# The start of a three-part attention and feed-forward kernel: the first block's loads, matrices, new states and layout put in another order

## The reference

```
# r, k, v: (batch 4, heads 8, seq 768, head_dim 48); w, u: (8, 48)
state = zeros(B, H, D, D)
for t in range(S):
    cur      = outer(u * k[t], v[t])
    y[t]     = r[t] @ (state + cur)
    state    = w * state + outer(k[t], v[t])
x = y arranged as (3072 tokens, 384)
h = relu(x @ w_in); x2 = (h * h) @ w_down            # 384 -> 2048 -> 384
out = ((x2 @ w_a) * (x2 @ w_b)) @ w_out              # 384 -> 1536 -> 384
```

## Time and profile before

| | |
|---|---|
| median of 3 runs | 972.02 us (970.56 to 972.78) |
| the profiled execution's own time | 973.94 us |
| its span | 972.2 us |
| TensorE busy (matmul) | 948.9 us, 98% of the span |
| VectorE, ScalarE, GpSimd busy | 398.8, 291.0, 129.4 us |
| granted TensorE clock, mean | 0.992 |

### The profile page before, as it was taken

How to read it: one execution, slowest core, us unless ns; L and a number is a source line. 1 busy time by engine, 2 the same in 40 slices (tenths; PEclk the granted TensorE clock), 3 DMA queues, 4 the chain that set the end, 5 groups by cost and what they waited for, 6 DMA issues and landing times.

```text
span 972.2 us, 16724 instructions
## 1 busy us (share of the span) xinstructions
PE 948.9 (98%) x7231; PEld 802.3 (83%) x7231; DVE 398.8 (41%) x571; ACT 291.0 (30%) x499; POOL 129.4 (13%) x124
## 2 busy tenths in 40 slices
PE   7899999999999999999999999999999999999997
PEld 6777787888788888888888888888888888888886
DVE  5378755556545636443563222222222222222221
ACT  2343432333333233324553222222222222222221
POOL 5235333224222403100000000000000000000000
PEclk9799999999999999999999999999999999999999
DMA  9454636203221430001431002002002001000001
GB/s 147 85 115 102 117 91 108 50 18 80 31 55 48 53 65 34 19 17 66 122 98 65 1 1 65 0 1 66 1 1 65 1 1 40 27 1 20 13 1 33
DMA packets 105688, 46.71 MB, mean 48 GB/s; under 512 B 78221, under 2 KB 104078, under 8 KB 105614
## 3 DMA queue, kind: packets, MB, share of 16 engines
q1 hardware_dynamic: 92048, 39.34, 18.4%
q10 hardware_dynamic: 13566, 6.30, 3.0%
HBM read 32.25 MB, written 9.44 MB: 43 GB/s over the span
## 4 chain that ended last, share of the span: by engine, by line
PE 93%; issue 2%; DVE 1%; ACTq 1%; ACT 1%; DMA 0%; POOL 0%; DVEq 0%; POOLq 0%
PE banks L711 10%; PE banks L712 10%; PE banks L710 10%; PE banks L604 8%; PE banks L605 7%; PE banks L608 7%; PE banks L588 6%; PE banks L589 6%; PE banks L590 6%; PE banks L726 5%; PE banks L725 5%; PE banks L729 5%; PE banks L535 2%; PE banks L478 2%; PE banks L503 1%
## 5 line engine op out<-in xcount | busy, mean ns | idle before, releaser
L1086 DVE TENSOR_TENSOR g_raw<-banks,g_raw 128x512 f32<-128x512 f32 x72 | 49.8, 692 | 284.6 <-PE banks L712 284.6
L711 PE MATMUL banks<-xT,weights 128*128 128x512 f32 x360 | 141.3, 393 | 0.0
L712 PE MATMUL banks<-xT,weights 128*128 128x512 f32 x360 | 141.1, 392 | 0.0
L710 PE MATMUL banks<-xT,weights 128*128 128x512 f32 x360 | 140.4, 390 | 0.0
L1007 DVE TENSOR_TENSOR g_lo<-g_raw,g_hi 128x512 fp32r<-128x512 f32 x96 | 81.9, 854 | 112.1 <-ACT g_hi L756 112.1
L604 PE MATMUL banks<-g_hi,weights 128*128 128x512 f32 x288 | 118.7, 412 | 0.0
L588 PE MATMUL banks<-xT,weights 128*128 128x512 f32 x288 | 113.0, 392 | 3.2 <-DVE weights L310 2.9
L605 PE MATMUL banks<-g_hi,weights 128*128 128x512 f32 x288 | 112.7, 391 | 0.0
L756 ACT ACTIVATE g_hi<-g_raw 128x512 fp32r<-128x512 f32 x96 | 60.7, 633 | 172.9 <-PE banks L608 162.9
L589 PE MATMUL banks<-xT,weights 128*128 128x512 f32 x288 | 112.3, 390 | 0.0
L590 PE MATMUL banks<-xT,weights 128*128 128x512 f32 x288 | 112.3, 390 | 0.0
(11 more groups left out here) (119 smaller groups left out, 1306.2 us busy)
## 6 DMA issues: line engine op xcount, KB each, us to landing
x_dram<-x SPq DMA_DIRECT2D x6, 768.0 KB, 3.2
xT<-x_dram SPq DMA_DIRECT2D x6, 768.0 KB, 5.2
rkv<-in_v SPq DMA_DIRECT2D x22, 192.0 KB, 5.2
result<-x SPq DMA_DIRECT2D x20, 192.0 KB, 2.9
stage<-in_moe_w_out SPq DMA_DIRECT2D x15, 192.0 KB, 3.0
xT<-y_pad SPq DMA_DIRECT2D x20, 144.0 KB, 2.7
stage<-in_moe_w_out ACTq DMA_DIRECT2D x13, 192.0 KB, 2.7
rkv<-in_k SPq DMA_DIRECT2D x12, 192.0 KB, 3.9
```

The lines of the kernel that those rows point to most:

```text
L710: nc.tensor.matmul(dst, hi, xT[:, q, HI, kt, :], start=(kt == 0), stop=False)
L711: nc.tensor.matmul(dst, hi, xT[:, q, LO, kt, :], start=False, stop=False)
L712: last = nc.tensor.matmul(dst, lo, xT[:, q, HI, kt, :], start=False, stop=(kt == KT - 1))
```

## The change

The change rewrites the order of the first block only; the loops over the later blocks stay. In words:

- SP issues the loads of `k` and `r` of the first half, then of the second, then both loads of `v`, then weight tiles 0 and 1. Before, SP issued `k`, `k`, `v` of the first half and the weight tiles, and ACT issued `r`, `r`, `v` of the second half and weight tile 2. ACT now issues only the loads of `w` and `u` at the start.
- SP then issues `repack(sp, 0)`, the six DMAs that lay out y of units 0 and 1, waits until all four units of y are gathered (`y_mixed` at 4), and only then issues weight tiles 2 and 3 and the loads of units 4 to 7.
- The diagonal matrices: units 0 and 2 on ACT, unit 1 on VectorE (one instruction), unit 3 on GpSimd.
- GpSimd starts `k_times_u` after VectorE's tables are made (`tables_made`), not when `u_rows` are there.
- TensorE: `renew_state` of units 0 and 1 stands after the gathering of y of both units and after `take_y` of its unit; `place_x` is called for units 2 and 3 only. 12 warming transposes in two groups of 6 take the place of 8 in one.
- `take_y` of unit 2 and 3 waits for the landed `repack(0)`, which reads the `y_pad` columns that it overwrites. `x_hi` and `x_lo` of units 0 and 1 read the landed copies.

```
--- before.py
+++ after.py
...
     RKV = 2 * (2 * RK + DM) + HP - D
     RK_LOADS, V_LOADS = 16 * 3, 16 * 2
     HI, LO = 0, 1
-    WARM_START, WARM_TURNS = 8, 8
+    WARM_START, WARM_TURNS = 8, 6
     assert B == 4 and BT == 512 and H * D == DM and KT == PAIRS - 1
     assert 2 * RKV >= LATE * 2 * W2 and (N2 - LATE) * 2 * W2 <= N1 * 2 * W1
...
         def placed(e):
-            return bank[UNITS + e][:, 0:DM].rearrange("p (k t) -> p k t", k=KT)
+            return bank[2 + e][:, 0:DM].rearrange("p (k t) -> p k t", k=KT)
+        def matrix_of(e):
+            return (eye[:, :].unsqueeze(1).unsqueeze(1).broadcast_to([P, 2, PAIRS, T]),
+                    diag[:, e % 2, :, :].rearrange("p g q -> p q g").unsqueeze(3).broadcast_to([P, 2, PAIRS, T]))
         x2_dram = nc.dram_tensor("x2_dram", [BLOCKS, P, KT * BT], F32, kind="Internal").ap()
         in_main = w_in[0:KT * MAIN, :].rearrange("(k p) f -> p k f", k=KT)
...
         scored, masked = sem("scored"), sem("masked")
         w_turned, u_spread, u_made = sem("w_turned"), sem("u_spread"), sem("u_made")
         diag_made, pad_made = sem("diag_made"), sem("pad_made")
-        matrices_made, last_matrix_made = sem("matrices_made"), sem("last_matrix_made")
+        matrices_made, odd_matrices_made = sem("matrices_made"), sem("odd_matrices_made")
         scores_ready, y_mixed, mixed = sem("scores_ready"), sem("y_mixed"), sem("mixed")
         ku_made, rku_made, k_tail_made = sem("ku_made"), sem("rku_made"), sem("k_tail_made")
         decay_made, state_made, state_read = sem("decay_made"), sem("state_made"), sem("state_read")
...
             return min(e, LEAVING)
         def half_landed(eng, e):
-            eng.wait_ge(x_landed[e // 2 % 2], REPACK * (e // UNITS))
+            eng.wait_ge(x_landed[e // 2 % 2], REPACK * (e // UNITS + (1 if e % UNITS < 2 else 0)))
         def half_loaded(eng, loaded, e):
             eng.wait_ge(loaded[e // 2 % 2], (V_LOADS if loaded is v_loaded else RK_LOADS) * (e // UNITS + 1))
...
                 sp.dma_start(xT[:, n % 2, LO, :, :].rearrange("p k t -> p (k t)").bitcast(F32),
                              x2_dram[n, :, :]).then_inc(x2_loaded[n % 2], 16)
-            load_rk(sp, 0, 1, k, k_loaded)
-            load_rk(sp, 2, 1, k, k_loaded)
-            load_v(sp, 0)
+            for e in (0, 2):
+                load_rk(sp, e, 1, k, k_loaded)
+                load_rk(sp, e, 0, r, r_loaded)
+            for e in (0, 2):
+                load_v(sp, e)
             load_weights(sp, 0)
             load_weights(sp, 1)
+            repack(sp, 0)
+            sp.wait_ge(y_mixed, UNITS)
+            load_weights(sp, 2)
+            load_weights(sp, STAGES)
             load_half(UNITS)
-            load_weights(sp, STAGES)
             load_half(UNITS + 2)
             for n in range(BLOCKS):
...
                     diag[:, e % 2, :, :].rearrange("p g q -> p q g").unsqueeze(3)
                     .broadcast_to([P, 2, PAIRS, T]), ALU.mult).then_inc(pad_made, 1)
+            def odd_matrix(e):
+                pool.wait_ge(diag_made, e + 1)
+                nc.gpsimd.tensor_tensor(pad_early[e], *matrix_of(e), ALU.mult).then_inc(odd_matrices_made, 1)
             pool.wait_ge(u_made, 1)
+            pool.wait_ge(tables_made, 1)
             for e in range(2):
                 k_times_u(e)
             for e in range(2):
                 times_r(e)
-            pool.wait_ge(pow_raw_made, 1)
             nc.gpsimd.tensor_tensor(tail_pow_t, pow_raw[:, :, ::-1],
                                     w_pow2[:, 5, :, :].rearrange("p g i -> p (g i)").unsqueeze(2)
                                     .broadcast_to([P, 2 * PAIRS, T]), ALU.mult).then_inc(tail_pow_made, 1)
...
                 k_times_u(e)
             pool.wait_ge(tail_made, 1)
             tail(0)
-            tail(1)
             for e in range(2, UNITS):
                 times_r(e)
-            pool.wait_ge(diag_made, UNITS)
-            nc.gpsimd.tensor_tensor(
-                pad_early[3], eye[:, :].unsqueeze(1).unsqueeze(1).broadcast_to([P, 2, PAIRS, T]),
-                diag[:, 1, :, :].rearrange("p g q -> p q g").unsqueeze(3).broadcast_to([P, 2, PAIRS, T]),
-                ALU.mult).then_inc(last_matrix_made, 1)
+            tail(1)
+            odd_matrix(3)
             tail(2)
             tail(3)
             decay(2)
...
             def first_scores(e):
                 half_loaded(pe, v_loaded, e)
                 pe.wait_ge(masked, e + 1)
-                if e < UNITS - 1:
-                    pe.wait_ge(matrices_made, e + 1)
-                else:
-                    pe.wait_ge(last_matrix_made, 1)
+                pe.wait_ge((matrices_made, odd_matrices_made)[e % 2], e // 2 + 1)
                 mix_scores(e)
             def place_x(e):
...
                 pe.wait_ge(y_made, e + 1)
                 cols = slice(e % 2 * P, (e % 2 + 1) * P)
                 for kt in range(KT):
-                    to = bank[UNITS + e][:, kt * P:(kt + 1) * P]
+                    to = bank[2 + e][:, kt * P:(kt + 1) * P]
                     nc.tensor.matmul(to, choose_own[0:PR], y_pad[0:PR, kt, cols], start=True, stop=False)
                     last = nc.tensor.matmul(to, choose_last[kt][0:PR], y_pad[0:PR, KT, cols], start=False, stop=True)
                 last.then_inc(x_placed, 1)
...
             turn_r(0)
             turn_r(1)
+            pe.wait_ge(u_made, 1)
+            free = [bank[1][:, j * P:(j + 1) * P] for j in range(4)]
+            warm(WARM_TURNS, free)
             pe.wait_ge(table_step, 1)
             turn_k(2)
             turn_k(3)
+            warm(WARM_TURNS, free)
             score(0)
+            score(1)
+            turn_r(2)
             pe.wait_ge(tail_pow_made, 1)
             for g in range(PAIRS):
                 last = nc.tensor.transpose(bank[3][:, g * P:(g + 1) * P],
                                            g_flat[:, BT + g * P:BT + (g + 1) * P], ident[:, :])
             last.then_inc(tail_turned, 1)
-            score(1)
-            pe.wait_ge(u_made, 1)
-            warm(WARM_TURNS, [bank[1][:, j * P:(j + 1) * P] for j in range(4)])
-            turn_r(2)
             pe.wait_ge(tail_made, 1)
             turn_r(3)
-            for e in range(2):
-                first_scores(e)
-                renew_state(e)
+            first_scores(0)
+            first_scores(1)
+            pe.wait_ge(y_made, 1)
+            renew_state(0)
             score(2)
             score(3)
             mix_state(2)
+            pe.wait_ge(y_made, 2)
+            renew_state(1)
             first_scores(2)
+            mix_state(3)
+            first_scores(3)
             pe.wait_ge(choice_made, 3)
-            place_x(0)
-            mix_state(3)
-            place_x(1)
-            first_scores(3)
             place_x(2)
             place_x(3)
             for e in range(2, UNITS):
                 renew_state(e)
             up(0, 0)
...
             def take_y(e):
                 act.wait_ge(y_mixed, e + 1)
-                if UNITS + 2 > e >= 2:
-                    act.wait_ge(x_placed, e - 1)
+                if UNITS <= e < UNITS + 2:
+                    act.wait_ge(x_placed, e - UNITS + 1)
                 elif e >= 2:
                     half_landed(act, e - 2)
-                if e < LEAVING and not 2 <= e < UNITS:
+                if UNITS <= e < LEAVING:
                     act.wait_ge(mixed, e + 1)
                 y = both(banks_of(e), 0, PAIRS * T)[0:PR].rearrange("p i (g t) -> p i g t", g=PAIRS)
                 to = y_pad[0:PR, :, e % 2 * P:(e % 2 + 1) * P].rearrange("p g (i t) -> p i g t", i=2)
                 nc.scalar.activation(to, y, ACT.Copy).then_inc(y_made, 1)
             def first_x_hi(e):
-                act.wait_ge(x_placed, e + 1)
+                act.wait_ge(x_placed, e - 1)
                 nc.scalar.activation(xT[:, 0, HI, :, cols_of(e)], placed(e), ACT.Copy).then_inc(x_hi_made, 1)
             def x_hi(e):
...
             act.dma_start(w_rows.rearrange("g (q d) -> g q d", q=2)[:, :, 0:D], w.rearrange("(g q) d -> g q d", q=2))\
                 .then_inc(w_loaded, 16)
             act.dma_start(u_row.rearrange("p (h d) -> p h d", h=H), u.unsqueeze(0)).then_inc(u_loaded, 16)
-            load_rk(act, 0, 0, r, r_loaded)
             act.wait_ge(u_spread, 1)
             nc.scalar.activation(u_rows[:, :, :].rearrange("p h d -> p (h d)"), bank[1][:, 0:DM], ACT.Copy)\
                 .then_inc(u_made, 1)
-            load_rk(act, 2, 0, r, r_loaded)
-            load_v(act, 2)
-            load_weights(act, 2)
-            act.wait_ge(tail_turned, 1)
-            nc.scalar.activation(tail_pow[:, :, :], bank[3][:, :].rearrange("p (h d) -> p h d", h=H)[:, :, 0:D],
-                                 ACT.Copy).then_inc(tail_made, 1)
             def make_matrices(e):
                 act.wait_ge(diag_made, e + 1)
                 for h in range(H):
...
             act.wait_ge(masks_made, 6)
             make_matrices(0)
```

(49 more changed lines are left out.)

## The result

The changed kernel took 966.24 us in the median of 4 executions (964.5 to 966.75), the kernel before 972.4 (970.56 to 973.01). The ratio is 0.9937, with a 95% interval of 0.9918 to 0.9955: 6.1 us less. Six more executions of it, measured later, had a median of 965.44 against 972.84 for 17 of the kernel before: 0.992 (0.9901 to 0.9939), 7.4 us less. The direction was as forecast; the forecast was 961.5, a gain of 10.5, with a range that ended at 965.5. The time lies 0.7 us outside it.

The account below looks back on a forecast made before the run. TensorE bounds, so `up(0, 0)` starting earlier is the gain: 5.8 + 1.4 + 1.8 + 1.0 (earlier start) + 0.5 (shorter gaps) = 10.5, taking 973.94 to 963.4, 961.5 as median. Range 959.5 to 963.5; 8 in 10, 957.5 to 965.5.

Parts of the forecast that it names:

- The tables at 0.69 each: VectorE's two table products: with GpSimd held back, 0.69 us each instead of 1.37 and 1.48.
- the chain through mask, sum, matrices and `tail_pow`: From `score(0)` at 14.1 through VectorE and ScalarE: `first_scores(0)` at 19.2 instead of 20.21, gaining only 1.0 us.
- the 150 GB/s of the forecast: Rate assumed for the early loads in one queue: `v` lands at 16.9 and 19.5, weight tiles by 24.
- 44.82 - 34.3 = 10.5: Start of `up(0, 0)` before, less its forecast start after: the whole gain, 10.5 us.
- One of the two issue waits stays, 1.0, and the one under the loads goes, since these now wait: TensorE between the first gatherings and `place_x(2)`: one wait of 1.0 us left, ending the second road at 30.0.
- the issue wait 1.8: Term of the sum: 1.8 us saved by losing the idle wait in `first_scores(2)`, during which loads ran.
- the rival to which I gave 0.10 at 964.5: Clock falls to 0.50 on the placing, which costs 3.0 us more: gain 7.5, 964.5 us; chance 0.10.
- two `place_x` at low clock 5.8: Term of the sum: dropping the placing of units 0 and 1 from TensorE saves 5.8 us.
- the low clock on what stood between and behind them 1.4: Term of the sum: work between and behind the two dropped placings escapes the low clock, saving 1.4 us.
- The waits for weights in the first steps stay as they were: Behind `up(0, 0)`, layer one: weight tile 2 lands at 34.5, just in time for its split; no added wait.
- The rival on the slower side: Held-back loads of units 4 and 5 starve layer one: 981 us at 50 GB/s; chance 0.03.
- The better rival: Before `up(0, 0)`, clock and queue run better, without issue waits: gain 13 to 14, 958.5 us; chance 0.25.

Follow-up runs that it names:

- again_2: The changed kernel with no edit, one single execution for a third trace: 966.61 us, no ratio.
- fill: The changed kernel with 14 more warming transposes ahead of the turning of `tail_pow`: 965.65 us, ratio 0.9926 to the kernel before.
- sums_first: The changed kernel with VectorE's diagonal sums of units 0 and 1 and unit 1's matrix ahead of unit 0's mask: 964.74 us, ratio 0.9915.
- pool_wait: The changed kernel with GpSimd starting `k_times_u(4)` only when the rest of weight tile 3 is made: 964.89 us, ratio 0.9912.
- pool_early: The changed kernel with GpSimd started when `u_rows` are there, beside VectorE's tables, as before: 965.84 us, ratio 0.992.
- more_code: The changed kernel with 32 tiny 4-column transposes in front of the turning of `tail_pow`, where TensorE waits: 966.63 us, ratio 0.9928.
- place_all: The changed kernel with `place_x` on TensorE for all four units and no `repack(0)`: 966.99 us, ratio 0.9937.
- again: The changed kernel with no edit, executed six more times: 965.44 us median, ratio 0.992 to the kernel before.
- again_3: The changed kernel with no edit, one single execution for a fourth trace: 964.9 us, no ratio.
- best_a: The changed kernel without the 12 warming transposes and with GpSimd's `k_times_u(4)` held until weight tile 3's rest is made: 963.03 us, ratio 0.9892.
- best_b: As best_a, with the sums of units 0 and 1 ahead of the mask as well: 962.18 us, ratio 0.9885.
- no_warm: The changed kernel without its 12 warming transposes (`WARM_TURNS` from 6 to 0): 962.94 us, ratio 0.9891.

## Why the prediction was wrong

**Right.** What bounds the kernel, and that all hangs on the start of `up(0, 0)`: the rest is 927.1 to 927.7 in six of the eight traces of the two kernels, 928.2 and 928.8 in two. The tables at 0.69 each, hidden; the matrix on VectorE (1.19 us) hidden; the chain through mask, sum, matrices and `tail_pow`, which put `first_scores(0)` at 19.2 (19.4 in the mean of four traces); loads of `r` near 9. The loads themselves were faster than the 150 GB/s of the forecast: 143 to 199 in stretches of 2 us between 5 and 17, through the one queue. That cost the forecast nothing, since no gathering waited for `v`.

**The step that failed** is the sum "44.82 - 34.3 = 10.5", at both ends: the mean start moved by 8.3.

The larger error is the start after, 34.3 against a mean of 35.74, 1.4 us. Up to `first_scores(0)` it is 0.2, and from `place_x(2)` to `up(0, 0)` another 0.2 (4.5 us and not 4.3). The other 1.1 lies between, where 10.8 us were forecast and 11.2 to 11.4 measured in three traces, 13.7 in again_2. The text there says "One of the two issue waits stays, 1.0, and the one under the loads goes, since these now wait". It was the other way round: the wait in the middle of `first_scores(2)`, the one under the loads, stayed in all four traces, with 1.14 to 2.23 us, though the loads were held back; the one in the scores was gone in three of four and 0.46 in the fourth. So 1.6 us of such waits are left in the mean and not 1.0. All waits for "issue" together fell by 1.8 in the mean (3.4 to 1.6), which is the sum's term "the issue wait 1.8"; with its reason, the loads, unsupported, that is luck. The rest is again_2's clock at 0.50 on the last gathering and the placing, the rival to which I gave 0.10 at 964.5. On the placing it held in one of four traces of the changed kernel; fill, sums_first, pool_wait, pool_early and more_code show it too.

The base is 0.8 too high. I measured the change from 44.82, a start that held 9.85 us of low clock; the starts before are 42.36 to 45.36, mean 44.04, since the low stretch ends at 36 in one execution and at 41 in another. The terms "two `place_x` at low clock 5.8" and "the low clock on what stood between and behind them 1.4" count that clock as part of what the change removes. At full clock the two placings cost 3.0 us, by place_all's trace. Then the full 10.5 was taken from the median: "the profiled execution has 973.94, 1.9 above the median; 963.4 there is 961.5 as a median".

**The third error** is "The waits for weights in the first steps stay as they were": 0.4 us in the mean, and against the first trace 1.5 in again and 0.8 in again_3, because the held-back load of unit 4 released GpSimd's product onto VectorE's products there. The Trainium skill, "SBUF — State Buffer", section "Summary: rules for kernel authors", says that the two block each other; I had weighed that on the tables and the matrix only. The traces agree: 1.75 us instead of 0.95 in again, 1.50 instead of 0.69 in again_3.

Together 0.8, 1.4 and 0.4 are 2.6, and 10.5 less 2.6 is the 7.9 of the means, near the 7.4 of the larger measurement. The four executions of each kernel that the forecast was held against give 6.2; the other 1.2 is their scatter. So is the side of the bound: the later median, 965.44, lies just inside the range that ended at 965.5.

**The rival on the slower side** (starved layer one) found nothing: the wait there was for VectorE, not for a load. **The better rival** (958.5) had "no issue wait at all" as a condition. No trace met it, and in fill and sums_first the waits grew as TensorE came sooner.

What stays open: why the wait in `first_scores(2)` is 1.1 us in one execution and 2.2 in another, what sets the time between pieces of code, and whether an extra load beside them costs anything.

## What to carry to other kernels

Before taking a difference from one trace, read where its low-clock stretches lie and ask whether a second execution would have them; a base read off an unlucky execution makes every change look better than it is. In a stretch of very small matmuls count the instructions: when a shortened chain only lengthens the waits for "issue", and these sit at fixed counts, the arrival of the code is the likely bound. Test warming transposes by leaving them out: the 12 here cost 2.5 us, while 14 more inside a wait (fill) cost nothing that could be measured. When loads are moved, look at which compute instruction their landing releases and what it then meets; the meeting can fall on another instruction in the next execution.

## What the runs showed of the hardware

The record of the granted clock says 1.00 from the start, but the first 128-column transposes took 0.20 us or more each and later ones 0.12 to 0.13: the warming transposes of the changed kernel at 11.20 (six in 1.28 us) and at 14.11 (six in 0.75). That is about the relation of the two levels as `place_x` shows it, also with 128 columns (0.43 us for two at 0.50, 0.22 at 1.00), so the early ones ran at the pace of 1.2 GHz, whatever the record says. When the pace changes differs between executions: in best_a eight transposes from 10.68 took 0.98, in more_code six from 13.99 still took 1.42. With the landing of `r` (9.00 to 9.45) it moves `score(0)` of the changed kernel between 13.36 and 14.86. No run shows that warming brings the change forward: without it, it came before 10.7 in best_a and not before 14 in best_b.

The clock also fell later, in most traces, and stayed at 0.50 for 3 to 10 us although TensorE then had little or no gap left. It fell inside an idle stretch of 1.2 to 2.5 us or up to 2.6 us behind one; but idle stretches of 2.36 and 1.53 us in no_warm, and of 1.40 in the changed kernel, left it at 1.00.
